# Tile sums ahead of the step's square on VectorE, and preparation work moved away from the tile boundaries, in an attention kernel with two gated layers

## The reference

```python
def _attn_ref(u, v, z):                 # u, v: (2, 3008, 256), z: (2, 3008, 64)
    scale = 1.0 / S                     # S = 3008
    scores = scale * np.matmul(z, z.transpose(0, 2, 1))
    attn = np.maximum(scores, 0.0) ** 2
    out = np.matmul(attn, v)
    return (u * out).astype(np.float32)
...
x = attn_out.reshape(B * S, D)          # 6016 tokens of 256
h = x @ w_in                            # 256 to 2048
x = (h - np.tanh(h)) @ w_out            # 2048 to 256
gate = 1.0 / (1.0 + np.exp(-(x @ w_gate)))   # 256 to 1536
val = x @ w_val
return (gate * val @ w_out)             # 1536 to 256
```

## Time and profile before

| | |
|---|---|
| median of 3 runs | 1523.26 us (1522.93 to 1525.82) |
| profiled execution, its own time | 1523.28 us |
| its span, first to last instruction | 1521.5 us |
| busy in it: TensorE, VectorE, ScalarE | 1498.3, 1135.1, 948.0 us |
| transfers | 241.79 MB, mean 159 GB/s |

### The profile page before, as it was taken

The page is one execution under the profiler, slowest core; times in us unless marked ns, Lnnn a source line. Parts: engine busy times, 40 slices in busy tenths (PEclk is TensorE's granted clock), DMA queues, the critical chain, the costliest instruction groups (busy, mean ns, idle before and its releaser), DMA issues.

```text
span 1521.5 us, 21890 instructions
## 1 busy us (share of the span) xinstructions
PE 1498.3 (98%) x8802; PEld 1320.1 (87%) x8802; DVE 1135.1 (75%) x1409; ACT 948.0 (62%) x1282; POOL 0.7 (0%) x5
## 2 busy tenths in 40 slices
PE   8999999999999999999999999999999999999998
PEld 7899998999999788888888888888888888888897
DVE  8888888889988676867777777766666676666655
ACT  7666666766666566666666666655555555555654
POOL 0000000000000000000000000000000000000000
PEclk9999999999999999999999999999999999999999
DMA  4433323154431435454544546544544545454352
GB/s 132 157 146 146 119 85 90 63 222 160 188 118 65 165 142 207 147 179 148 184 159 155 180 156 236 209 143 180 193 174 180 187 168 198 181 182 186 132 208 87
DMA packets 36325, 241.79 MB, mean 159 GB/s; under 512 B 3584, under 2 KB 6656, under 8 KB 22912
## 3 DMA queue, kind: packets, MB, share of 16 engines
q1 hardware_dynamic: 36080, 240.17, 43.3%
q10 hardware_dynamic: 144, 0.23, 0.0%
HBM read 196.21 MB, written 44.17 MB: 158 GB/s over the span
## 4 chain that ended last, share of the span: by engine, by line
PE 95%; DVE 3%; ACT 1%; issue 0%; POOLq 0%; DVEq 0%; ACTq 0%
PE acc L455 24%; PE hidden L409 12%; PE hidden L411 12%; PE hidden L410 12%; PE acc L409 10%; PE acc L410 10%; PE acc L411 10%; PE hidden L432 5%; DVE part_lo L785 1%; DVE h L891 1%; ACT part_hi L710 1%; DVE x_out L837 0%; PE acc L563 0%; DVE h L854 0%; ACT snap L650 0%
## 5 line engine op out<-in xcount | busy, mean ns | idle before, releaser
L785 DVE TENSOR_TENSOR part_lo<-h,part_hi 128x1024 fp32r<-128x1024 f32 (+2 forms) x315 | 375.0, 1191 | 111.8 <-ACT part_hi L710 61.0
L455 PE MATMUL acc<-part_hi,region 64*128 64x512 f32 (+1 forms) x2256 | 406.1, 385 | 13.9 <-DVE x_out L837 11.3
L650 ACT ACTIVATE snap<-hidden 128x512 f32<-128x512 f32 (+1 forms) x360 | 211.8, 588 | 254.0 <-PE hidden L411 253.7
L409 PE MATMUL hidden<-region 128*128 128x512 f32 (+1 forms) x840 | 324.9, 387 | 2.6 <-ACT snap L650 1.9
L410 PE MATMUL hidden<-region 128*128 128x512 f32 (+1 forms) x840 | 324.2, 386 | 0.0
L411 PE MATMUL hidden<-region 128*128 128x512 f32 (+1 forms) x840 | 324.1, 386 | 0.0
L455 PEld LDWEIGHTS acc<-part_hi,region 64*128 64x128 f32 x2256 | 269.6, 185 | 23.5 <-issue 15.7
L854 DVE TENSOR_TENSOR h<-hidden,snap 128x512 f32<-128x512 f32 (+1 forms) x252 | 170.9, 678 | 148.8 <-ACT snap L650 122.4
L455 PE MATMUL acc<-part_lo,region 64*128 64x512 f32 (+1 forms) x1128 | 260.5, 384 | 0.0
L409 PE MATMUL acc<-part_hi,region 128*128 128x512 f32 (+1 forms) x672 | 259.6, 386 | 0.2 <-DVE part_lo L785 0.2
L410 PE MATMUL acc<-part_lo,region 128*128 128x512 f32 (+1 forms) x672 | 259.4, 386 | 0.0
(11 more groups left out here) (56 smaller groups left out, 1197.9 us busy)
## 6 DMA issues: line engine op xcount, KB each, us to landing
region<-ready SPq DMA_DIRECT2D x33, 2304.0 KB, 9.0
region<-ready SPq DMA_DIRECT2D x51, 1408.0 KB, 6.2
ready<-region SPq DMA_DIRECT2D x6, 2304.0 KB, 7.6
ready<-region SPq DMA_DIRECT2D x8, 1408.0 KB, 5.6
xs<-x_out SPq DMA_DIRECT2D x20, 512.0 KB, 5.5
x_in<-xs SPq DMA_DIRECT2D x20, 512.0 KB, 7.9
snap<-vP SPq DMA_DIRECT2D x24, 256.0 KB, 2.7
u_in<-uT SPq DMA_DIRECT2D x10, 512.0 KB, 5.3
```

Of the source, the lines that this page charges most:

```text
L409: pe.matmul(dst, w_hi, x_hi, start=start, stop=False, skip_group_check=True)
L455: last = pe.matmul(acc[:, 2 * r + d, 0:w], v[ROWS[r], 2 * p + c, half], a[ROWS[r], 2 * (s % 2) + c, 0:w], start=start, stop=False, skip_gr ...
L650: act.activation(snap[:, g % 2, i, 0:w], hidden[:, CHAIN[g % 2], 0:w], ACT.Copy).then_inc(s_snap, 1)
L785: return ve.tensor_tensor(dst, whole, hi.bitcast(F32), ALU.subtract)
```

## The change

- In a step of `GATE_AT`, VectorE does the tile sums ahead of that step's square, no longer behind it; the product with u goes one step later, and the tile's store and the next load of u with it.
- The weight pieces get a table of steps of their own: 15 + 6 k and the three behind it for the first layer; for the second, the steps from 81 on that are neither a boundary step nor the one behind it.
- The z tasks of the second batch go to steps 19, 31, 43, 55, 63 and 65, its v tasks to steps 67 to 80 without 73 and 74, and the x pieces to 131, 132 and 135 to 139.
- At the start z piece 1 is split in step 0, ahead of the relu. The two halves of step 0 are done one after the other (relu, square, `part_lo`), no longer stage by stage. There is one pair of warm-up matmuls less.

```diff
-WARM = 9
+WARM = 8
...
-    tasks = [(max(0, 2 * k - 1), "z", (0, k)) for k in range(ZP)]
-    tasks += [(AT[0, p], "v", (0, p)) for p in range(STEPS)]
-    tasks += [(AT[TPB - 1, 2 * k], "z", (1, k)) for k in range(ZP)]
-    tasks += [(AT[TPB, 0] + p - 2, "v", (1, p)) for p in range(STEPS)]
+    tasks = [(0, "z", (0, 0)), (0, "v", (0, 0)), (0, "z", (0, 1))]
+    tasks += [(2 * k - 1, "z", (0, k)) for k in range(2, ZP)]
+    tasks += [(p, "v", (0, p)) for p in range(1, STEPS)]
+    tasks += [(at, "z", (1, k)) for k, at in enumerate((19, 31, 43, 55, 63, 65))]
+    later = [at for at in range(67, 81) if at not in GATE_AT and at - 1 not in GATE_AT]
+    tasks += [(at, "v", (1, p)) for p, at in enumerate(later)]
     return sorted(tasks, key=lambda t: t[0])
...
-WSTART = tuple(12 + 6 * k for k in range(UNITS[0])) + tuple(82 + 7 * k for k in range(UNITS[1]))
...
-X0_LOAD, X0_SUMS, X0_SPLIT = 125, 127, 131
+def weight_steps():
+    free = [s for s in range(81, 125) if s not in GATE_AT and s - 1 not in GATE_AT]
+    for k, pieces in enumerate(WPIECES):
+        if WLAYER[k] == 0:
+            yield tuple(15 + 6 * k + i for i in range(2 + pieces))
+        else:
+            yield tuple(free.pop(0) for _ in range(2 + pieces))
+
+
+WSTEPS = tuple(weight_steps())
+WEIGHTS_AT = {s: (k, i) for k, steps in enumerate(WSTEPS) for i, s in enumerate(steps)}
+X0_LOAD, X0_SUMS = 125, 127
+X0_SPLIT = (131, 132, 135, 136, 137, 138, 139)
...
                 for T in range(NT - 1):
-                    if s == GATE_AT[T] + 1:
+                    if s == GATE_AT[T] + 2:
                         store_tile(T)
                         load_u(T + 1)
                 for k in range(len(WLAYER)):
-                    if s == WSTART[k] - 3:
+                    if s == WSTEPS[k][0] - 3:
                         load_raw(k)
-                    if s == WSTART[k] + 2 + WPIECES[k]:
+                    if s == WSTEPS[k][-1] + 1:
                         store_prepared(k)
...
                 if s == 0:
                     for c in range(2):
                         act.wait_ge(s_score, c + 1)
                         act.activation(first[:, 0, c, 0:w], hidden[:, c, 0:w], ACT.Relu,
                                        scale=1.0 / SEQ).then_inc(s_relu, 1)
-                    for c in range(2):
                         act.wait_ge(s_relu, c + 1)
                         act.activation(part_hi[:, c, 0:w], first[:, 0, c, 0:w],
                                        ACT.Square).then_inc(s_ahi, 1)
...
-                for task in tasks_at(s, "z"):
+                for task in tasks_at(s):
                     split_task(task)
+                if s in GATE_AT:
+                    sum_halves(GATE_AT.index(s))
                 if s == 0:
                     for c in range(2):
                         ve.wait_ge(s_relu, c + 1)
                         ve.tensor_tensor(full[:, 0, c, 0:w], first[:, 0, c, 0:w],
                                          first[:, 0, c, 0:w], ALU.mult).then_inc(s_full, 1)
-                    for task in tasks_at(s, "v"):
-                        split_task(task)
-                    for c in range(2):
                         ve.wait_ge(s_full, c + 1)
                         ve.wait_ge(s_ahi, c + 1)
                         minus(part_lo[:, c, 0:w], full[:, 0, c, 0:w],
                               part_hi[:, c, 0:w]).then_inc(s_alo, 1)
                     continue
-                for task in tasks_at(s, "v"):
-                    split_task(task)
                 ve.wait_ge(s_relu, behind(s))
                 ve.tensor_tensor(full[:, k, :, 0:w], first[:, k, :, 0:w], first[:, k, :, 0:w],
                                  ALU.mult).then_inc(s_full, 1)
-                if s in GATE_AT:
-                    sum_halves(GATE_AT.index(s))
...
-                if s in GATE_AT:
-                    gate_by_u(GATE_AT.index(s))
+                if s - 1 in GATE_AT:
+                    gate_by_u(GATE_AT.index(s - 1))
```

More of the change, by code:

```diff
@@ L131 @@
 TASK_NUMBER = {(kind, i): k for k, (_, kind, i) in enumerate(TASKS)}
+assert len(TASKS) == 2 * (ZP + STEPS)
+assert all(TASKS[TASK_NUMBER["v", (1, p)]][0] >= AT[TPB - 1, p] + 2 for p in range(STEPS))
+assert all(TASKS[TASK_NUMBER["v", (1, p)]][0] <= AT[TPB, p] for p in range(STEPS))
 WLAYER = (0,) * UNITS[0] + (1,) * UNITS[1]
-WSTART = tuple(12 + 6 * k for k in range(UNITS[0])) + tuple(82 + 7 * k for k in range(UNITS[1]))
 WPIECES = tuple((2, 4)[la] for la in WLAYER)
 WPIECES_BEFORE = tuple(sum(WPIECES[:k]) for k in range(len(WLAYER) + 1))
-X0_LOAD, X0_SUMS, X0_SPLIT = 125, 127, 131
-assert max(WSTART) + 6 < X0_LOAD and X0_SPLIT + 7 <= NSTEP
+def weight_steps():
[9 more added lines that the diff above has]
+X0_SPLIT = (131, 132, 135, 136, 137, 138, 139)
+assert max(WEIGHTS_AT) < X0_LOAD
 def build(nc, uT, zT, vP, w1, w2, out):
@@ L240, in build, with tasks_at @@
         block = ctx.enter_context(nc.Block())
-        def tasks_at(s, kind):
-            return [k for k, task in enumerate(TASKS) if task[:2] == (s, kind)]
+        def tasks_at(s):
+            return [k for k, task in enumerate(TASKS) if task[0] == s]
         def staged(k):
@@ L262, in weight_step @@
         def weight_step(s):
[L265 to L268, removed]
+            return WEIGHTS_AT.get(s, (None, None))
         def weight_blocks(k):
@@ L682, in _ @@
                 w, k = tile_width(T), s % 2
-                for task in tasks_at(s, "z") + tasks_at(s, "v"):
+                for task in tasks_at(s):
                     split_task(task)
@@ L702, in _ @@
                     split_weights(unit, i - 2)
-                if X0_SPLIT <= s < X0_SPLIT + 7:
-                    split_x(0, s - X0_SPLIT)
+                if s in X0_SPLIT:
+                    split_x(0, X0_SPLIT.index(s))
                 if s in GATE_AT:
```

## The result

| | before | changed |
|---|---|---|
| median of 4 runs, us | 1523.28 (1522.93 to 1525.82) | 1509.49 (1509.01 to 1510.14) |
| profiled execution, its span | 1523.28, 1521.5 | 1509.4, 1507.6 |

What follows compares the result with a forecast made beforehand. TensorE bounds the kernel, waiting for VectorE's tile sums. Gains 6.23 + 1.14 + 1.26 + 1.50 + 1.69 + 1.1 = 12.92, less 0.2, take 1523.28 to 1510.6 us; own range 1508.5 to 1512, whole range 1507.5 to 1515.5.

Steps and rivals of the forecast that it cites:

- What bounds it: TensorE, busy 98%, waits at tile boundaries for VectorE's tile sums, queued behind an unneeded square: eleven times, 11.3 us.
- Sums ahead of the square: At tile boundaries the sums start earlier: 0.89 at seven, 1.14 at the first, 1.26 for two before 448-token tiles.
- What becomes late in its place: Behind a boundary, the next square and `part_lo` follow the sums, yet stay hidden with 0.53 to spare.
- lower bound's mechanism: At a boundary, the second copy holds the sums until today's end; each boundary would keep 0.53 instead of 0.89.
- Moved preparation: Weight and z pieces go to steps without a boundary, the gate product one step later; moves costed at nothing.
- wait comes back as a wait for `part_lo`: Rival: VectorE doesn't catch up behind a boundary, so TensorE waits a few steps later; 1520.5 us, chance 0.07.
- The boundary between the batches and the clock: At step 73, without the v task, sums start earlier for 1.50; full clock in attend(72) returns 1.69.
- the drop would come elsewhere: Rival: TensorE's clock drop stays or hits another gap; 1512.3 us, chance 0.17.
- The first step: At the start, `part_lo` of the first half follows its square at once: 1.1 gained, bounds 0.24 and 1.36.
- Transfers: x load costs 0.2 (bounds 0 to 2.1), unit stores unseen; rival of late transfers 1512.5 to 1516, chance 0.13.
- the 1.5 that the forecast named as a sign against it: In the profile after, VectorE should show no wait for the x load over 1.5 us.
- slack of 1.47: Delay of `part_lo` in a step that TensorE doesn't see: 1.47 us, used for unit stores and the x load.

Runs made afterwards that it cites:

- e1_sums_behind: The changed kernel with the tile sums behind the step's square again, all moved preparation and the new first step kept: 1519.46 us.
- e7_copy_first: The changed kernel with nine warm-up pairs and, in boundary steps, ScalarE's first copy ahead of the relu, the second behind it: 1511.99 us.
- e5_first_step_only: The kernel before with only the new first step and one warm-up pair less: 1520.36 us.
- e6_x_sum_early: The changed kernel with the first x sum one step earlier, 126 instead of 127: 1513.35 us.
- e3_warm9: The changed kernel with nine warm-up pairs instead of eight: 1509.90 us.
- e4_old_first_step: The changed kernel with the old first step (halves stage by stage, z piece 1 in step 1, v piece between, nine warm-up pairs): 1511.77 us.
- e2_sums_only: The kernel before with the tile sums ahead of the square as the only edit: 1521.89 us.

## Why the prediction held, and where it was thin

- *What bounds it.* Right: the sums' wait was TensorE's, the square ahead of them was the cause, and with that order back 10 us return (`e1_sums_behind`).
- *Sums ahead of the square.* Right in mechanism, small in size: 0.95 on average for 0.89 at the seven like boundaries. The sum starts 0.03 behind the copy, where I allowed the 0.09 of another handover. Behind tile 0 it was 1.38 for 1.14, from two sources: the sums came 0.95 earlier against `part_lo`, as elsewhere, and `part_lo` itself came 0.41 earlier against ScalarE's square. Before, that square ended at 49.79 and `part_lo` started at 50.30; now they meet at 48.95 and 49.05. What held `part_lo` for that 0.41 before isn't shown. The forecast gave the whole of its 1.14 to the square's duration.
- *What becomes late in its place.* `part_lo` behind the sums ended 0.45 ahead of the next attend. Less the handover of 0.14, as in the forecast, 0.31 is left of the 0.53 worked out there. The sum counted 1.28 for two sums in a row, and the second one waited for the second copy (1.49). So the lower bound's mechanism is there, but too small to reach TensorE; in `e7_copy_first` it reaches it.
- *Moved preparation, "I cost these moves at nothing".* Right as a term, and the thinnest place of the reasoning. The forecast took each boundary's 0.89 as the gain of the order and the moves as free. In fact the order alone gives 1.4. With the new order, the weights' move is worth 4.7, and the product's 2.5 more beside the old weights. The rival "wait comes back as a wait for `part_lo`" is what the kernel without the moves does; that the moves prevent it, which the rival's "against" said in one line, decides most of the result: the order is worth 10.0 with them and 1.4 without.
- *The boundary between the batches and the clock.* 3.19 as forecast, in other shares: the clock gave 1.6, the boundary 1.6. The rival that the drop would come elsewhere isn't seen in the profiled run, and the three others lie within 0.8 of it. But the term is no fixed price of that gap: `e5_first_step_only` keeps the gap and mostly pays nothing. The profile of before from which the 1.69 was read had the drop, and the median measured against, 1523.28, is that execution's time; that let the term come out whole, and here the forecast was lucky.
- *The first step.* Too large, 0.83 for 1.1. `part_lo` of the first half started at 7.55, not 7.3, because the relu ended later: the scores ran at 1.2 GHz for longer (their twelve matmuls took 1.94 instead of 1.55). The moment at which the clock rose differed by over 2 us between executions of kernels whose warm-up starts alike, and the gain of the same new first step ran from 0.52 to 1.11 over nine profiles.
- *Transfers.* The x load was hidden (0.02), though VectorE waited 1.60 for it, just over the 1.5 that the forecast named as a sign against it. ScalarE waited for a unit's store at two places, 0.64 and 0.40, inside the 0 to 1 of the forecast, and TensorE didn't see it; `e6_x_sum_early` shows that the slack of 1.47 in that term was real.
- *The last 0.57.* What lies between the last score step and the end of the attention was not in the sum, and the other profiles speak against counting it to the change. In the trace of before, matmuls of scores and attends overlap in the records of the last steps, near 492 us, as if the two row halves had drifted apart; from the scores at 474.03 to the layers' first matmul at 500.39 it takes 26.36. In the changed kernel there is no such overlap, and the same stretch, 460.63 to 486.43, takes 25.80. Six of the fourteen profiles have no overlap there and take 25.77 to 25.80, among them `e5_first_step_only`, whose boundaries are those of before. The others overlap, and where the same scores can be told in the records they take 26.21 to 26.36, among them `e3_warm9`, which differs from the changed kernel by one warm-up pair. So this gain came with the profiled execution; without it the profiles differ by 13.4.
- *Open.* What sets the overlap off isn't shown. Why both old places together cost 7.2 and not the expected 9.2 is also not settled.

## What to carry to other kernels

Where the bounding engine waits for an operation that stands behind one not needed yet, swapping the two is only half of the change: add up all the other engine's work in the next two or three steps against their deadlines, since the wait returns there if the queue can't drain. Test a reordering without the moves that accompany it before crediting either. Count a clock drop behind a gap as something that happens in part of the executions; only a gap that is gone is sure to cause none.

## What the hardware showed that was not expected

- The same gap of TensorE, 1.69 us, was followed by 1.2 GHz in one profile of a kernel (1522.06), while its nine other runs, at a mean granted clock of 1.000, were 1.6 to 2.2 us shorter; a gap of 2.61 at the start was followed by full clock in the profile of before and by 1.2 GHz in that of `e4_old_first_step`.
- Two operations of VectorE of which the second reads nothing of the first overlap by 0.09 in the records (93.82 + 1.22 against 94.95 in `e2_sums_only`), while a `part_lo` that waits for the square just ahead starts 0.03 behind its end (92.22 + 1.22 against 93.47 in the changed kernel): in these rows a dependence costs about 0.1 us even on one engine.
- Score and attend matmuls overlap in the records of the attention's last steps in eight of the fourteen profiles and not in the six others, and the stretch takes some 0.5 us longer with it (26.21 to 26.36 against 25.77 to 25.80).
